# Attention with keys on partitions: row maxima from a first pass put as six rows under the queries

## The chip, the core and the metric

The kernel runs on one core of a Trainium2 chip. The metric is the device time of one execution in microseconds. The engines of a core are TensorE (PE, matrix products into PSUM), VectorE (DVE), ScalarE (ACT), GpSimd (POOL) and SyncE (SP, which issues transfers). Each takes its own instructions in order and they meet only at semaphores.

## The reference

```python
scores = scale * np.matmul(q, k.transpose(0, 1, 3, 2))
scores = np.where(mask, scores, -1000000000.0)
scores = scores - np.max(scores, axis=-1, keepdims=True)
attn = np.exp(scores)
attn = attn / (np.sum(attn, axis=-1, keepdims=True) + 1e-09)
return np.matmul(attn, v).astype(np.float32)
```

There are 2 batches of 8 heads with 768 queries and keys of 64 dimensions, all f32. `mask` is true where a query and a key have the same nearest centroid of 16. The heads' outputs side by side are 1,536 rows of 512, which go through a dense layer pair (512 to 2,048 to 512, with a gate) and then through a top-2 mixture of 8 experts. The change is in the attention part alone.

## The kernel before

Attention takes the first third of the time. The 16 heads (`HEADS`) go in pairs, the middle pairs in a hardware loop, with `x` from 0 to 11 over the pair's tiles of 128 queries (`J` = 6 to a head). For each tile TensorE runs, two tiles ahead, `scores`: 128 queries by 768 keys in two halves of 384 columns, each half a product of the high parts `qa`, `ka` and one of the low parts `qb`, `kb`. Under the 64 dimensions of `qa` and `ka` lie 16 rows that hold the cluster of each query and key, so that the product carries the mask. Two pairs of PSUM banks take the scores in turn. VectorE takes the maximum of a tile (`row_max`), ScalarE the exponential with that maximum as bias (`exps`). The probabilities have queries on partitions, so TensorE transposes them, six blocks of 128 (`turn_probs`), VectorE and ScalarE each copy half of them back (`probs_t`), and `values` multiplies them with the values and a column of ones (`vx`, 65 columns) in plain f32. After six tiles VectorE divides by the denominators (`head_result`, over 6 columns), and after a pair `turn_pair` transposes the result into the layout `xt_hi`, `xt_lo` that the dense layer reads.

Once a head the clusters are found: `similarity` on TensorE, `similarities` and `clusters` on VectorE, `turn_onehot` on TensorE, `cluster_rows` on ScalarE. Bank 7 serves these one after the other (`prep_ready`, `prep_free`). `rows` splits the loaded queries and keys into high and low parts, ScalarE the high and VectorE the low. GpSimd scales the queries and copies the values beside the ones. SyncE loads two heads ahead. What an engine does when is written out by hand in the order of the code. Names of the changed kernel that have a namesake keep its task.

## Time and profile before

| | |
|---|---|
| runs, us | 979.66, 977.3, 978.07 (median 978.07) |
| profiled execution, us | 980.6, of it the span of instructions 978.9 |
| busy, us (share of the span) | PE 928.0 (95%), DVE 535.7 (55%), ACT 407.0 (42%), POOL 115.3 (12%) |
| first product of the dense layers starts at, us | 323.46 |

Matmuls overlap in the pipeline, so the busy time of TensorE says that it has work, not how fast it works; prices are read from distances between starts. A row such as `L719 PE MATMUL psum<-vx,probs_t 128*128 128x65 f32 x12` is twelve records of line 719 with 128x128 weights and 65 moving columns.

### The profile page before, as it was taken

To read this page: it belongs to the slowest core of one execution; us is meant where nothing else is said; L and a number is where in the kernel's file an instruction comes from. 1 tells how busy PE (TensorE), PEld (TensorE's weight loads), DVE (VectorE), ACT (ScalarE), POOL (GpSimd) and SP (SyncE) were. 2 spreads that over 40 slices of the span, in tenths; PEclk is the share of its full clock that TensorE was granted. 3 is DMA by queue.
4 is the path that set the end of the run, shared out by engine and by line. 5 is a ranking of instruction groups with operands and counts; after the bars stand their busy time and mean duration, and the time that the engine had idled before them with its cause. 6 is when DMAs were issued, how large, how long until landed. Compare 5 with 4: busy or idle time off the path is not lost.

```text
span 978.9 us, 15299 instructions
## 1 busy us (share of the span) xinstructions
PE 928.0 (95%) x5483; PEld 826.9 (84%) x5483; DVE 535.7 (55%) x995; ACT 407.0 (42%) x589; POOL 115.3 (12%) x123
## 2 busy tenths in 40 slices
PE   2999999999999999999999996499999999999995
PEld 2999999999999888888888885388888888888884
DVE  4477787787786644355443644254343444435374
ACT  3455665665665522234333422134343342434320
POOL 3010010010010000000500140500000000004162
PEclk9999999999999999999999998599999999999998
DMA  7014214214520522333523342534342634537364
GB/s 208 1 42 125 83 40 123 83 40 123 164 91 1 172 86 100 114 105 113 173 87 127 105 152 86 162 130 154 136 161 86 204 97 153 179 107 244 131 214 156
DMA packets 74052, 118.88 MB, mean 121 GB/s; under 512 B 6970, under 2 KB 37690, under 8 KB 74016
## 3 DMA queue, kind: packets, MB, share of 16 engines
q1 hardware_dynamic: 69088, 104.08, 33.0%
q0 software_dynamic: 4928, 14.35, 4.2%
q8 instruction: 20, 0.33, 0.1%
q14 instruction: 16, 0.13, 0.0%
HBM read 89.12 MB, written 29.39 MB: 121 GB/s over the span
## 4 chain that ended last, share of the span: by engine, by line
PE 94%; DVE 2%; DMA 1%; ACT 1%; POOL 1%; issue 1%; SPq 1%; POOLq 0%; DVEq 0%
PE psum L719 13%; PE psum L777 10%; PE psum L779 10%; PE psum L778 10%; PE psum L791 9%; PE psum L793 9%; PE psum L792 9%; PE psum L709 7%; PE psum L696 4%; PE psum L697 4%; PE psum L925 2%; PE psum L672 2%; PE psum L789 1%; PE psum L788 1%; PE psum L881 1%; PE psum L684 1%
## 5 line engine op out<-in xcount | busy, mean ns | idle before, releaser
L791 PE MATMUL psum<-down_hi,hid_hi 128*128 128x512 f32 x384 | 151.3, 394 | 0.0
L792 PE MATMUL psum<-down_lo,hid_hi 128*128 128x512 f32 x384 | 149.8, 390 | 0.0
L793 PE MATMUL psum<-down_hi,hid_lo 128*128 128x512 f32 x384 | 149.8, 390 | 0.0
L719 PEld LDWEIGHTS psum<-vx,probs_t 128*128 128x128 f32 x1152 | 143.6, 195 | 0.1
L719 PE MATMUL psum<-vx,probs_t 128*128 128x65 f32 x1152 | 141.3, 273 | 0.0
L982 ACT ACTIVATE probs<-psum,neg_max 128x768 f32<-128x768 f32 x96 | 86.5, 901 | 91.6 <-DVE neg_max L1219 91.2
L1114 ACT ACTIVATE hid_hi<-psum 128x448 fp32r<-128x448 f32 x64 | 34.8, 544 | 185.5 <-PE psum L779 185.4
L1474 DVE SCALAR_TENSOR_TENSOR hid_lo<-psum,hid_hi 128x384 fp32r<-128x384 f32 x64 | 35.6, 556 | 123.9 <-ACT hid_hi L1114 123.9
L1219 DVE TENSOR_REDUCE neg_max<-psum 128x1 f32<-128x768 f32 x96 | 91.6, 954 | 16.9 <-PE psum L697 16.9
L777 PE MATMUL psum<-sx_hi,up_hi 128*128 128x448 f32 x256 | 94.7, 370 | 0.0
L778 PE MATMUL psum<-sx_lo,up_hi 128*128 128x448 f32 x256 | 94.4, 369 | 0.0
L779 PE MATMUL psum<-sx_hi,up_lo 128*128 128x448 f32 x256 | 94.3, 368 | 0.0
L1089 ACT ACTIVATE gelu<-psum 128x512 f32<-128x512 f32 x48 | 28.7, 598 | 157.4 <-PE psum L779 157.4
L1242 DVE TENSOR_TENSOR up_lo<-raw,up_hi 128x1024 fp32r<-128x1024 f32 x56 | 68.5, 1223 | 40.6 <-ACT down_hi L1003 40.5
L793 PEld LDWEIGHTS psum<-down_hi,hid_lo 128*128 128x128 f32 x384 | 72.1, 188 | 15.4
L791 PEld LDWEIGHTS psum<-down_hi,hid_hi 128*128 128x128 f32 x384 | 72.1, 188 | 14.6 <-DVE hid_hi L1474 0.2
L709 PE MATMUL psum<-ident,probs 128*128 128x128 f32 x576 | 83.4, 282 | 0.9 <-ACT probs L982 0.7
L792 PEld LDWEIGHTS psum<-down_lo,hid_hi 128*128 128x128 f32 x384 | 72.1, 188 | 13.9
L1258 DVE COPY probs_t<-psum 128x384 f32<-128x384 f32 x96 | 53.3, 555 | 46.6 <-PE psum L709 45.6
L1424 DVE CAST hid_hi<-gelu 128x512 fp32r<-128x512 f32 x48 | 20.8, 432 | 105.5 <-ACT gelu L1089 105.5
L696 PE MATMUL psum<-ka,qa 80*128 80x384 f32 x192 | 75.2, 392 | 1.7 <-ACT ka L977 1.7
L777 PE MATMUL psum<-xt_hi,up_hi 128*128 (+1 forms) x192 | 76.3, 398 | 0.0
(181 smaller groups left out, 1549.1 us busy)
## 6 DMA issues: line engine op xcount, KB each, us to landing
raw<-in_moe_w SPq DMA_DIRECT2D x64, 512.0 KB, 4.3
raw<-in_moe_w_in SPq DMA_DIRECT2D x24, 512.0 KB, 3.4
raw<-in_moe_w_out SPq DMA_DIRECT2D x24, 512.0 KB, 5.1
slot_x<-zeros SPq DMA_DIRECT2D x7, 1024.0 KB, 5.6
raw_q<-in_q SPq DMA_DIRECT2D x32, 192.0 KB, 3.3
raw_k<-in_k SPq DMA_DIRECT2D x32, 192.0 KB, 3.7
slot_rows<-slot_x SPq DMA_DIRECT2D x8, 768.0 KB, 5.4
slot_y<-y_sb SPq DMA_DIRECT2D x7, 768.0 KB, 3.9
```

Of the source, the lines that this page charges most:

```text
L696: mm(dst, qa[0:D + C, s, cols], ka[0:D + C, s, keys], start=True, stop=False)
L709: last = nc.tensor.transpose(psum[:, 4 + half, j * P:(j + 1) * P], src, ident[:])
L719: last = mm(psum[:, 6, i * VW:(i + 1) * VW], probs_t[:, i % 2, j // 3, (j % 3) * P:(j % 3 + 1) * P], vx[:, s, j], start=(j == 0), stop=(j ...
L777: mm(dst, up_hi[:, slot, c, cols], moving_hi(c), start=(c == 0), stop=False)
L778: mm(dst, up_hi[:, slot, c, cols], moving_lo(c), start=False, stop=False)
L779: last = mm(dst, up_lo[:, slot, c, cols], moving_hi(c), start=False, stop=(c == DC - 1))
L791: mm(dst, hid_hi[:, f % 2, cols], down_hi[:, slot, f % GP], start=(f == 0), stop=False)
L792: mm(dst, hid_hi[:, f % 2, cols], down_lo[:, slot, f % GP], start=False, stop=False)
L793: return mm(dst, hid_lo[:, f % 2, cols], down_hi[:, slot, f % GP], start=False, stop=(f == pieces - 1))
L982: copy(probs[:, i % 2].rearrange("p (h n) -> p h n", h=2), src, ACT.Exp, bias=neg_max[:, i % 2:i % 2 + 1]).then_inc(probs_ready, 1)
L1219: dv.tensor_reduce(neg_max[:, i % 2:i % 2 + 1], psum[:, 2 * (i % 2):2 * (i % 2) + 2, 0:HALF], AX.XY, ALU.max, negate=True).then_inc(max_re ...
L1242: dv.tensor_tensor(up_lo[:, slot], raw1[:, stage], up_hi[:, slot].bitcast(F32), ALU.subtract)
```

## The change

The scores of the probabilities are computed with keys on partitions, so that they need no transposing before the product with the values.

- **First pass.** `scores` runs the product of the high parts alone, for one head ahead, into one pair of banks. `row_max` writes the negated maximum of each tile into a column of `neg_max`. After six tiles `turn_max` transposes these columns into 6 rows of 128, and `max_to_rows` writes them as six rows of 768 under the queries of `qa`, each row zero outside its own tile. `ka` has ones in the same six rows, so the second pass subtracts the maximum of each query within the product.
- **Second pass.** A head is 12 units (`UNITS`): two halves of 384 queries, six blocks of 128 keys each. `turned` makes the scores of a unit in two products, two units ahead, in three banks; `exps` takes the exponential; `values` multiplies them in plain f32 with 128 stationary columns, 64 of the values and 64 of ones, and 386 moving columns. Its result has dimensions on partitions for the head's own half and the denominators on the other half.
- **Result.** `denominators` on ScalarE copies the denominators beside the results, `head_result` on VectorE inverts 64 x 384 of them and multiplies, twice a head. `pair_hi` on ScalarE copies that to `xt_hi`, GpSimd subtracts for `xt_lo`. The copies `probs_t`, `turn_probs` and `turn_pair` are gone; so is GpSimd's work on queries and values. The scale is applied in the exponential, the values are loaded in place.
- **Order.** `qa`, `ka`, `qb`, `kb` have three slots, loads are three heads ahead, `raw_q` and `raw_k` one slot. The attention is written out head by head, without loops. The dense layer starts when the first half of the last head is ready.

```diff
-            def load_head(n, s):
+            def load_rows(n):
                 for dst, src in ((raw_q, q_h), (raw_k, k_h)):
                     for half in range(2):
-                        sp.dma_start(dst[half * D:(half + 1) * D, s],
-                                     src[bass.ds(n, 1)].rearrange("o d n -> d (o n)")).then_inc(qk_in[s], DMA)
-                sp.dma_start(raw_v[:, s], v_h[bass.ds(n, 1)].rearrange("o p n -> p (o n)")).then_inc(v_in[s], DMA)
+                        sp.dma_start(dst[half * D:(half + 1) * D], src[n]).then_inc(qk_in, DMA)
+            def load_values(n):
+                sp.dma_start(vx[:, n % 2, :, own(n)], v_h[n]).then_inc(v_in[n % 2], DMA)
...
+            xt_flat = xt_hi[:].rearrange("p c n -> p (c n)"), xt_lo[:].rearrange("p c n -> p (c n)")
+            for n in range(1, HEADS, 2):
+                for half in range(2):
+                    pool.wait_ge(pair_hi_ready, n + half)
+                    hi, lo = (x[:, x_columns(n, half)] for x in xt_flat)
+                    nc.gpsimd.tensor_tensor(lo, head_x[:, half], hi.bitcast(F32), ALU.subtract)\
+                        .then_inc(pair_lo_ready, 1)
...
-            def scores(s, i, u):
+            def scores(m, i):
                 if i == 0:
-                    pe.wait_ge(prep_free, u)
-                p = i % 2
-                cols = slice(i * P, (i + 1) * P)
+                    pe.wait_ge(prep_free, prep[f"turn {m}"] + 1)
+                if m or i:
+                    pe.wait_ge(max_ready, J * m + i)
                 for half in range(2):
-                    keys = slice(half * HALF, (half + 1) * HALF)
-                    dst = psum[:, 2 * p + half, 0:HALF]
-                    mm(dst, qa[0:D + C, s, cols], ka[0:D + C, s, keys], start=True, stop=False)
-                    last = mm(dst, qb[:, s, cols], kb[:, s, keys], start=False, stop=True)
+                    last = mm(psum[:, half, 0:HALF], qa[0:D + C, m % SLOTS, i * P:(i + 1) * P],
+                              ka[0:D + C, m % SLOTS, half * HALF:(half + 1) * HALF], start=True, stop=True)
                 last.then_inc(scores_ready, 1)
...
+            def turn_max(m, use, tiles):
+                pe.wait_ge(max_ready, J * m + tiles)
+                pe.wait_ge(prep_free, prep[use])
+                nc.tensor.transpose(psum[0:J, 7, 0:P], neg_max[:, m % 2], ident[:]).then_inc(prep_ready, 1)
+            def turned(n, u, rows_set=None):
+                half, c = divmod(u, J)
+                at = UNITS * n + u
+                if rows_set is not None:
+                    pe.wait_ge(max_rows, rows_set)
+                if at >= SLOTS:
+                    pe.wait_ge(probs_ready, at - SLOTS + 1)
+                dst = bank(2 + at % SLOTS)[:, 0:HALF]
+                keys, queries = slice(c * P, (c + 1) * P), slice(half * HALF, (half + 1) * HALF)
+                mm(dst, ka[0:ROWS, n % SLOTS, keys], qa[0:ROWS, n % SLOTS, queries], start=True, stop=False)
+                mm(dst, kb[:, n % SLOTS, keys], qb[:, n % SLOTS, queries], start=False, stop=True)\
+                    .then_inc(turned_scores, 1)
+            def values(n, u):
+                half, c = divmod(u, J)
+                at = UNITS * n + u
+                if u == 0:
+                    pe.wait_ge(v_in[n % 2], DMA * (n // 2 + 1))
+                if c == 0 and n:
+                    pe.wait_ge(head_out, 2 * (n - 1) + half + 1)
+                pe.wait_ge(probs_ready, at + 1)
+                mm(psum[:, 5 + half, 0:WIDE], vx[:, n % 2, c], probs[:, at % SLOTS], start=(c == 0),
+                   stop=(c == J - 1)).then_inc(unit_done, 1)
+            def ahead(n, u):
+                if u + 2 < UNITS:
+                    turned(n, u + 2, 2 if n == 0 and u + 2 == J else None)
+                elif n + 1 < HEADS:
+                    turned(n + 1, u + 2 - UNITS, n + 3 if u + 2 == UNITS else None)
...
+            def head(n):
+                for u in range(UNITS):
+                    ahead(n, u)
+                    values(n, u)
+                    if n + 1 < HEADS:
+                        if u in (0, 2, 4, 6):
+                            scores(n + 1, 2 + u // 2)
+                        elif u == 8:
+                            turn_max(n + 1, f"max {n + 1}", J)
+                    if n + 2 < HEADS:
+                        if u == 1:
+                            similarity(n + 2)
+                        elif u == 5:
+                            turn_onehot(n + 2)
+                        elif u in (8, 10):
+                            scores(n + 2, (u - 8) // 2)
...
+            def exps(n, u):
+                at = UNITS * n + u
+                act.wait_ge(turned_scores, at + 1)
+                if at >= SLOTS:
+                    act.wait_ge(unit_done, at - SLOTS + 1)
+                copy(probs[:, at % SLOTS, 0:HALF], psum[:, 2 + at % SLOTS, 0:HALF], ACT.Exp, scale=float(D) ** -0.5)\
+                    .then_inc(probs_ready, 1)
+            def denominators(n, half):
+                act.wait_ge(unit_done, UNITS * n + (half + 1) * J)
+                if n:
+                    act.wait_ge(head_out, 2 * (n - 1) + half + 1)
+                copy(recip[own(n), half], psum[other(n), 5 + half, 0:HALF], ACT.Copy, bias=1e-9)\
+                    .then_inc(denom_ready, 1)
...
-            def row_max(tile, i):
-                dve.wait_ge(scores_ready, tile + 1)
-                dv.tensor_reduce(neg_max[:, i % 2:i % 2 + 1], psum[:, 2 * (i % 2):2 * (i % 2) + 2, 0:HALF],
-                                 AX.XY, ALU.max, negate=True).then_inc(max_ready, 1)
-            def head_result(n, s, chain):
-                dve.wait_ge(pv_done, J * n + J)
-                o = psum[:, 6, 0:J * VW].rearrange("p (j w) -> p j w", w=VW)
-                chain.link(dv.tensor_scalar(denom[:], o[:, :, D:VW], 1e-9, None, ALU.add))
-                chain.link(dv.reciprocal(recip[:], denom[:]))
-                dv.tensor_tensor(pair_x[:, :, s * D:(s + 1) * D], o[:, :, 0:D], recip[:].broadcast_to((P, J, D)),
-                                 ALU.mult).then_inc(head_out, 1)
-            def pair_lo(g, half):
-                dve.wait_ge(pair_hi_ready, 2 * g + half + 1)
-                at = (g & (DC - 1)) * N + (g & DC) * (S // DC) + half * HALF
-                hi = xt_hi[:].rearrange("p c n -> p (c n)")[:, bass.ds(at, HALF)].bitcast(F32)
-                lo = xt_lo[:].rearrange("p c n -> p (c n)")[:, bass.ds(at, HALF)]
-                dv.tensor_tensor(lo, psum[:, 7, 0:HALF], hi, ALU.subtract).then_inc(prep_free, 1)
+            def row_max(m, i):
+                dve.wait_ge(scores_ready, J * m + i + 1)
+                dv.tensor_reduce(neg_max[:, m % 2, i:i + 1], psum[:, 0:2, 0:HALF], AX.XY, ALU.max, negate=True)\
+                    .then_inc(max_ready, 1)
...
+            def max_to_rows(m, use, first, count):
+                full = (J, count, P)
+                dve.wait_ge(prep_ready, prep[use] + 1)
+                dv.scalar_tensor_tensor(
+                    out=qa[TOP:ROWS, m % SLOTS, first * P:(first + count) * P].rearrange("r (j q) -> r j q", q=P),
+                    in0=psum[0:J, 7, 0:P].rearrange("r (o q) -> r o q", o=1).broadcast_to(full), scalar=LARGEST,
+                    in1=own_tile[0:J, first:first + count].rearrange("r (j o) -> r j o", o=1).broadcast_to(full),
+                    op0=ALU.min, op1=ALU.mult).then_inc(prep_free, 1)
+                dve.wait_ge(prep_free, prep[use] + 1)
+                dve.sem_inc(max_rows, 1)
+            def head_result(n, half):
+                rows, held = own(n), psum[own(n), 5 + half]
+                dve.wait_ge(denom_ready, 2 * n + half + 1)
+                if n >= 2:
+                    dve.wait_ge(pair_lo_ready, 2 * (n // 2 - 1) + half + 1)
+                chain.mark(dv.tensor_scalar(mean_v[rows, half:half + 1], held[:, HALF:HALF + 1], 1e-9 / S, None,
+                                            ALU.mult))
+                chain.link(dv.reciprocal(recip[rows, half], recip[rows, half]))
+                dv.scalar_tensor_tensor(out=head_x[rows, half], in0=held[:, 0:HALF], scalar=mean_v[rows, half:half + 1],
+                                        in1=recip[rows, half], op0=ALU.add, op1=ALU.mult).then_inc(head_out, 1)
...
+            def head(n):
+                if n + 2 < HEADS:
+                    rows(n + 2, 1)
+                if n + 1 < HEADS:
+                    row_max(n + 1, 2)
+                head_result(n - 1, 1)
+                if n + 2 < HEADS:
+                    similarities(n + 2)
+                if n + 1 < HEADS:
+                    row_max(n + 1, 3)
+                if n + 2 < HEADS:
+                    clusters(n + 2)
+                if n + 1 < HEADS:
+                    row_max(n + 1, 4)
+                    row_max(n + 1, 5)
+                head_result(n, 0)
+                if n + 1 < HEADS:
+                    max_to_rows(n + 1, f"max {n + 1}", 0, J)
+                if n + 2 < HEADS:
+                    row_max(n + 2, 0)
+                    row_max(n + 2, 1)
+                if n + 3 < HEADS:
+                    rows(n + 3, 0)
...
+            pe.wait_ge(pair_lo_ready, PAIRS)
+            pe.wait_ge(head_out, 2 * HEADS - 1)
+            chunk(0, None)
+            pe.wait_ge(pair_lo_ready, 2 * PAIRS)
```

The next two pieces are VectorE's order, first of a head in the loop of the kernel before, from the result of the head before it. `neg_max` is the maximum of a tile, `probs_t` the copy of its transposed half; lines 1210 to 1214 are `clusters`.

```order
L1225 TENSOR_SCALAR denom<-psum 128x6
L69 ISA
L1226 RECIPROCAL recip<-denom 128x6
L69 REGISTER_ALU
L1227 TENSOR_TENSOR pair_x<-psum,recip 128x6x64
L1201 ISA
L1203 TENSOR_REDUCE sim<-psum 128x192
L1257 ISA
L1258 COPY probs_t<-psum 128x384
L1218 REGISTER_ALU
L1219 TENSOR_REDUCE neg_max<-psum 128x1
```

In the changed kernel the same engine between the clusters of one head and the second result of that head, from `row_max` of tiles 4 and 5 on:

```order
L1294 TENSOR_REDUCE neg_max<-psum 128x1 x2
L1315 TENSOR_SCALAR mean_v<-psum 64x1
L1317 RECIPROCAL recip<-recip 64x384
L1318 SCALAR_TENSOR_TENSOR head_x<-psum,mean_v,recip 64x384
L1301 SCALAR_TENSOR_TENSOR qa<-psum,own_tile 6x768
L1294 TENSOR_REDUCE neg_max<-psum 128x1 x2
L1268 SCALAR_TENSOR_TENSOR qb<-qa,split_q,raw_q 128x768
L1268 SCALAR_TENSOR_TENSOR kb<-ka,split_k,raw_k 128x768
L1294 TENSOR_REDUCE neg_max<-psum 128x1
```

The result of a head stands twice in a head instead of once, with 384 columns instead of 6, and ahead of the six rows of maxima; the copies are gone.

On TensorE a tile of the kernel before reads (transposes of the probabilities, scores two tiles ahead, values of the tile before):

```order
L709 MATMUL psum<-ident,probs 128x128 x6
L696 MATMUL psum<-ka,qa 128x384
L697 MATMUL psum<-kb,qb 128x384
L696 MATMUL psum<-ka,qa 128x384
L697 MATMUL psum<-kb,qb 128x384
L719 MATMUL psum<-vx,probs_t 128x65 x6
```

and in the changed kernel units 8 to 10 of a head, with the scores of the first pass (line 707) between them; the product of line 727 at unit 10 is the first that reads the six rows:

```order
L727 MATMUL psum<-qa,ka 128x384
L728 MATMUL psum<-qb,kb 128x384
L740 MATMUL psum<-probs,vx 128x386
L715 MATMUL psum<-ident,neg_max 6x128
L707 MATMUL psum<-ka,qa 128x384 x2
L727 MATMUL psum<-qa,ka 128x384
L728 MATMUL psum<-qb,kb 128x384
L740 MATMUL psum<-probs,vx 128x386
L727 MATMUL psum<-qa,ka 128x384
L728 MATMUL psum<-qb,kb 128x384
L740 MATMUL psum<-probs,vx 128x386
L707 MATMUL psum<-ka,qa 128x384 x2
```

The six transposes and their products of 65 columns are replaced by one product of 386 columns a unit, and `neg_max` is turned between unit 8 and 9.

## Rows read from the trace of the kernel before

**Rows 1.** The page, part 4, shares of the chain that ended last.

```profile
PE 94%; DVE 2%; DMA 1%; ACT 1%; POOL 1%; issue 1%; SPq 1%; POOLq 0%; DVEq 0%
```

**Rows 2.** TensorE in order of time, 199 to 238 us: start, duration, line, names, form.

```profile
199.79 0.82 PE L672 MATMUL psum<-cen_r,qb 128*128 x6
...
220.57 1.45 PE L719 MATMUL psum<-vx,probs_t 128*128 128x65 f32 x12
221.85 0.82 PE L709 MATMUL psum<-ident,probs 128*128 128x128 f32 x6
222.43 0.42 PE L696 MATMUL psum<-ka,qa 80*128 80x384 f32 x1
222.69 0.34 PE L697 MATMUL psum<-kb,qb 128*128 128x384 f32 x1
222.87 0.34 PE L696 MATMUL psum<-ka,qa 80*128 80x384 f32 x1
...
224.60 0.62 PE L684 MATMUL psum<-ident_b,onehot 128*16 128x128 bf16 x12
...
236.48 0.82 PE L672 MATMUL psum<-cen_r,qb 128*128 x6
237.15 0.82 PE L672 MATMUL psum<-cen_r,kb 128*128 x6
```

**Rows 3.** All engines in order of time, the start of the attention part.

```profile
21.89 0.69 PE L696 MATMUL psum<-ka,qa 80*128 80x384 f32 x1 [1.71 <-ACT ka L977]
...
22.70 0.52 PE L696 MATMUL psum<-ka,qa 80*128 80x384 f32 x1
23.02 0.52 PE L697 MATMUL psum<-kb,qb 128*128 128x384 f32 x1
...
23.57 0.96 DVE L1219 TENSOR_REDUCE neg_max<-psum 128x1 f32<-128x768 f32 x1 [4.44 <-PE psum L697]
...
43.25 0.34 PE L697 MATMUL psum<-kb,qb 128*128 128x384 f32 x1
43.43 0.34 PE L696 MATMUL psum<-ka,qa 80*128 80x384 f32 x1
```

**Rows 4.** Groups of VectorE by line and form: busy us, mean ns, idle before.

```profile
L1219 DVE TENSOR_REDUCE neg_max<-psum 128x1 f32<-128x768 f32 x96 | 91.6, 954 | 16.9 <-PE psum L697 16.9
...
L1242 DVE TENSOR_TENSOR up_lo<-raw,up_hi 128x1024 fp32r<-128x1024 f32 x56 | 68.5, 1223 | 40.6 <-ACT down_hi L1003 40.5
...
L1258 DVE COPY probs_t<-psum 128x384 f32<-128x384 f32 x96 | 53.3, 555 | 46.6 <-PE psum L709 45.6
...
L1197 DVE SCALAR_TENSOR_TENSOR qb<-qa,split_q,raw_q 128x768 fp32r<-128x768 f32 x16 | 16.2, 1010 | 3.4 <-ACT qa L968 3.4
...
L1214 DVE TENSOR_TENSOR onehot<-iota_c,first_hit 128x192 bf16<-128x192 f32 x16 | 6.7, 420 | 0.6
...
L1213 DVE TENSOR_REDUCE first_hit<-hit 128x12 f32<-128x192 f32 x16 | 5.6, 353 | 0.6
```

**Rows 5.** Single lines of VectorE: ns min/median/max, first and last start.

```profile
L1184 DVE RECIPROCAL cen_s<-cen_s x1: 164/164/164, 6.0 to 6.0; 128x1 f32<-128x1 f32 x1
...
L1382 DVE RECIPROCAL r_t<-r_t x3: 178/178/178, 465.7 to 610.1; 128x4 f32<-128x4 f32 x3
...
L1226 DVE RECIPROCAL recip<-denom x16: 191/192/192, 53.4 to 323.9; 128x6 f32<-128x6 f32 x16
...
L1225 DVE TENSOR_SCALAR denom<-psum x16: 164/164/165, 53.2 to 323.7; 128x6 f32<-128x6 f32 x16
```

**Rows 6.** Two lines of TensorE with plain f32 products, same columns.

```profile
L719 PE MATMUL psum<-vx,probs_t x1152: 219/275/418, 33.2 to 323.4; 128*128 128x65 f32 x192
...
L881 PE MATMUL psum<-wr,yt x96: 177/263/263, 420.0 to 602.5; 128*128 128x16 f32 x96
```

**Rows 7.** Groups of ScalarE by line and form.

```profile
L1016 ACT ACTIVATE probs_t<-psum 128x384 f32<-128x384 f32 x96 | 46.5, 485 | 18.3 <-PE psum L709 18.1
...
L977 ACT ACTIVATE ka<-psum 16x768 fp32r<-16x768 bf16 x16 | 12.9, 803 | 0.2
```

More of the change, by code:

```diff
@@ L32 @@
 MASKED = 1e30
+LARGEST = 1e25
 CAP = 448
@@ L327, in rows_of @@
             return P if j < FULL else REST
-        def unit(g, k, first=False):
-            return 2 + k if first and k < 2 else 6 * g + k
+        prep = {}
+        for use in ("sim 0", "turn 0", "max 0", "max 0 again", "sim 1", "turn 1", "sim 2", "turn 2", "max 1"):
+            prep[use] = len(prep)
+        for n in range(1, HEADS):
+            for use, m in (("sim", n + 2), ("turn", n + 2), ("max", n + 1)):
+                if m < HEADS:
+                    prep[f"{use} {m}"] = len(prep)
         AT_LOGITS = TPC
@@ L767, in up @@
+            similarity(0)
+            turn_onehot(0)
+            for i in range(J // 2):
+                scores(0, i)
+            turn_max(0, "max 0", J // 2)
+            turned(0, 0, 1)
+            turned(0, 1)
+            for i in range(J // 2, J):
+                scores(0, i)
+            turn_max(0, "max 0 again", J)
+            first_head()
+            for n in range(1, HEADS):
+                head(n)
             def up(f, slot, moving_hi, moving_lo, width, group, turned_in=None):
@@ L1033, in _, with next_exps @@
[L1033 to L1043 removed]
+            def next_exps(n, u):
+                if u + 1 < UNITS:
+                    exps(n, u + 1)
+                elif n + 1 < HEADS:
+                    exps(n + 1, 0)
@@ L1044, in take_y @@
+            rows(0, 0)
+            rows(0, 1)
+            cluster_rows(0)
+            rows(1, 0)
+            rows(1, 1)
+            exps(0, 0)
+            first_head()
+            for n in range(1, HEADS):
+                head(n)
+            denominators(HEADS - 1, 1)
             def take_y(first):
@@ L1276, in _ @@
-            for n in range(2):
-                for w in range(2):
-                    rows(n, n, w)
-            similarities(0)
-            clusters(chain, 0)
-            row_max(0, 0)
-            row_max(1, 1)
-            pair(0, True, False, chain)
-            before_pairs = chain.n
-            PER_PAIR = 2 * 4 + 2 * 2
-            with dve.Fori(1, PAIRS - 1) as g:
-                body = Tally(dve, dve_chain, before_pairs + (g - 1) * PER_PAIR)
-                pair(g, False, False, body)
-                assert body.n == PER_PAIR
@@ L1290, in _, with first_head @@
-            chain = Tally(dve, dve_chain, before_pairs + (PAIRS - 2) * PER_PAIR)
-            pair(PAIRS - 1, False, True, chain)
-            head_result(HEADS - 1, 1, chain)
-            split(0, 1, 0)
-            split(0, 1, 1)
+            def first_head():
+                rows(1, 0)
+                rows(1, 1)
+                similarities(1)
+                clusters(1)
+                rows(2, 0)
+                rows(2, 1)
+                row_max(1, 0)
+                row_max(1, 1)
+                similarities(2)
+                row_max(1, 2)
+                clusters(2)
+                row_max(1, 3)
+                head_result(0, 0)
+                row_max(1, 4)
+                row_max(1, 5)
+                max_to_rows(1, "max 1", 0, J)
+                row_max(2, 0)
+                row_max(2, 1)
+                rows(3, 0)
@@ new lines, in _ @@
+            rows(0, 0)
+            rows(0, 1)
+            similarities(0)
+            clusters(0)
+            for i in range(J // 2):
+                row_max(0, i)
+            max_to_rows(0, "max 0", 0, J // 2)
+            for i in range(J // 2, J):
+                row_max(0, i)
+            max_to_rows(0, "max 0 again", J // 2, J // 2)
+            first_head()
+            for n in range(1, HEADS):
+                head(n)
+            for x in range(4):
+                split(0, x // 2, x % 2)
```

366 lines of the change are left out of this document (153 added, 213 removed).

## Prediction

> **What bounds the kernel now.** I read the chain of waits first. TensorE holds 94% of the chain that ended last [rows 1], so the question is what it issues in the attention part and whether anything stops it there. In the time-ordered rows of TensorE the same place of the loop (the two similarity groups) comes at 199.79 and at 236.48 us: a pair of heads takes 36.69 us, a head 18.35 us, and between those points TensorE stands without a gap [rows 2]. The reader should take prices from the distance of starts, because the durations overlap: six transposes of the probabilities 0.58 us (221.85 to 222.43), a product of 384 columns 0.18 us (222.69 to 222.87) or 0.26 us where it follows transposes (222.43 to 222.69), twelve value records 1.28 us (220.57 to 221.85), a similarity group of six 0.67 us (236.48 to 237.15), the twelve one-hot transposes about 0.6 us. A tile of 128 queries is then 0.58 + 0.26 + 3 x 0.18 + 1.28 = 2.66 us, and six tiles, 1.34 of similarity, 0.6 of one-hot and 0.33 of pair transposes make 18.2 of the 18.35 us. VectorE works beside it: per tile 0.954 us of maximum and a copy of 0.555 us [rows 4]. It has about 4 us of slack in a head.
>
> At the start products of 384 columns stand 0.32 us apart (22.70 to 23.02), and 0.18 us apart from 43.25 us on [rows 3]: 384 columns in 0.32 us are 1.2 GHz, so the tiles before that run at the lower clock and the rest at 2.4 GHz; I go by these distances, since the clock row of the page shows no drop there. The six value tiles of head 0 are done at 53.2 us, those of head 15 at 323.7 [rows 5].
>
> **What the change does to TensorE.** Per head it removes 36 transposes (6 x 0.58 = 3.5 us), 72 value records (6 x 1.28 = 7.7 us), half of the 24 score products of the first pass, and the pair transposes. It adds 12 units, each of two products of 384 columns (0.36 us) and one product of 386 columns in plain f32. The trace shows no wide f32 product. It does show that an f32 product is two records (1,152 for 576), and the shortest record goes from 177 ns at 16 columns to 219 at 65 [rows 6]: 42/49 = 0.86 ns a column, twice the 0.42 that one column takes at 2.4 GHz. So I take 386 x 0.86 = 0.33, with a little for issue 0.34 us a record and 0.67 a unit. From below, one record could cost 0.18 like the 384-column row; from above I allow double, 0.68. A unit is 0.36 + 0.67 = 1.03 us, and a head 12 x 1.03 + 12 x 0.18 (first pass) + 1.34 + 0.6 + 0.1 (turning the maxima) = 16.6 us. On TensorE alone the change gives 1.75 us a head.
>
> **What it does to VectorE.** Per head: six maxima 6 x 0.954 = 5.7 us, two splits of rows 2.0, sim 0.56, clusters 4 x 0.353 + 0.42 = 1.8, and no copies of probabilities any more [rows 4]. New is `max_to_rows`, six partitions by 768 elements: 1.0 us, like the 768-element row split. New too are two results a head: a tensor_scalar 0.16, a reciprocal over 64 x 384, and a multiplication of 384 columns 0.56, priced like the copy. The reciprocal is the disputed price. Before, it ran over 6 columns. Its three rows are 164 ns for 1 column, 178 for 4, 192 for 6, while the tensor_scalar of 6 columns takes 164 [rows 5]. End to end that is 28/5 = 5.6 ns a column, where ordinary operations pay about 1.05 (555 ns for 384, 954 for 768 [rows 4]). Over 384 columns: 0.16 + 383 x 0.0056 = 2.3 us. From below, if only the fixed part differs, 0.56 us as an ordinary operation of 384 columns; from above the steepest pair of rows, 7 ns: 2.84 us. I take 2.3, since sixteen repeats of the 6-column row spread by 1 ns. VectorE then has 5.7 + 2.0 + 0.56 + 1.8 + 1.0 + 2 x (0.16 + 2.3 + 0.56) = 17.1 us a head, over TensorE's 16.6.
>
> The Trainium skill, "VectorE: DVE Perf Modes", in the walkthrough of the 8-slice pipeline, says that a reciprocal is an iterated divide with a repeat count of 8. If that is 8 cycles a column at the page's 0.96 GHz, an estimate from that page is 3.35 us, and the sum below would end near 1,033 us; the three rows, 14 ns apart each, are flatter than that.
>
> **The ring of waits.** The two engines wait for each other, so I walked one head, with t = 0 where `max_to_rows` ends and about 0.05 us for each hand-over. TensorE stands at unit 10, whose first product reads those rows. It issues the unit (1.1 us, first product 0.26) and then `scores` of tile 1, which needs `row_max` 0 (done at 1.0): the scores are there at 1.8 (the last product runs 0.34 after its start). VectorE waits from 1.0 to 1.8, takes `row_max` 1 to 2.75, the row splits to 3.7 and 4.6, `row_max` 2 to 5.5, `head_result` of the previous half to 8.4, sim to 8.9, `row_max` 3 to 9.7, `clusters` to 11.6. TensorE, past its units 11 and 0 to 5, waits 0.4 us for the one-hot, turns it until 12.2, issues unit 6 and the scores of tile 5, done at 13.9. There is one pair of banks for the first pass, so VectorE waits from 12.5 (after `row_max` 4) to 13.9; that is the largest wait. `row_max` 5 ends at 14.9. ScalarE's cluster rows (2 x 0.8), one exponential and the denominator copy (0.485 each [rows 7]) end at 14.85, just in time. `head_result` takes 14.9 to 17.8, `max_to_rows` to 18.75. TensorE has reached unit 10 at about 17 and waits 1.7 us. Queued behind that waiting product are the values of unit 10 and the scores of the next head, which VectorE waits for: the ring closes at **18.75 us a head against 18.35**. ScalarE has 15 operations of 384 columns and 4 of 768 a head, 15 x 0.485 + 4 x 0.8 = 10.5 us [rows 7], and only queues.
>
> **The ends.** Start: scores of head 0 can begin at 21.9 as before [rows 3], since the longer chain of constants on VectorE takes back what the missing scaling on GpSimd gives. But then six times (scores 1.0 at the low clock, maximum 0.95) run one after the other, where before two buffers let tiles overlap; with two turns of the maxima, 1.0 us each, and two units between, unit 0 begins near 37 us. Head 0 holds two similarities, two clusterings and a result, with 1.93 us a unit until the clock rises near 55: the first `max_to_rows` of a full ring ends at 68.4, and head 0's twelve units at 70.9, against 53.2 before: +17.7. Thirteen rings: 13 x (18.75 - 18.35) = +5.2. End: head 14 without clusters needs 17.1 from ring to ring, then 2.5 + 12 x 1.03 = 14.9 to the last value at 68.4 + 243.75 + 17.1 + 14.9 = 344.2. VectorE has its last full result at 343.4 and two weight splits of 1.22 [rows 4] behind it, so the first layer starts at 345.8 instead of 323.46 and loses 1.0 in its second piece to the last `head_result`; it saves 0.65 of pair transposes. In all +22.7 us. The rest of the kernel moves as a block. The profiled execution took 980.6 (span 978.9): 1,003.3, and scaled to the median of the runs, 978.07/980.6, **1,001 us**.
>
> How it hangs on the reciprocal: 26 of them in the rings, one in head 0 and four at the end lie in the chain, so 0.1 us of its price is 3.1 us of the kernel. The sum breaks even at 2.3 - 22.7/31 = 1.57 us.
>
> **Rivals.** (1) *Cheap reciprocal, TensorE stays the bound; faster.* At 0.56 us VectorE has 13.6 us a head and the ring follows TensorE with about 16.8: 66.6 + 13 x 16.8 + 14.3 + 14.9 = 314.2, the first layer 9 us earlier in all: about 969. For it: the 10 ns between tensor_scalar and reciprocal at few columns might be fixed. Against it: 164, 178 and 192 rise with the columns. It decides for faster below 1.57 us. (2) *Steeper reciprocal:* 2.84 us gives 1,018; the pair 4 to 6 columns speaks for it, 1 to 4 against. The count of 8 in the Trainium skill's page (above) points the same way and further. (3) *The scores' hand-over is looser than my walk* (VectorE's next operation can begin some 0.08 before the last ends, and both engines may settle with less than 2.2 us of VectorE waiting): 1 us less in a ring is 985. (4) *Values at 0.68 us a record:* a unit of 1.7, a head of 24.7 on TensorE, 13 x 6 more, about 1,085. The 0.86 ns a column speaks against it. (5) *The ends alone:* if the clock rose during the first maxima, head 0 would be some 6 us shorter, 995; this lies in the forecast's own range and its chance in the forecast's.
>
> **How the numbers follow.** Forecast (reciprocal 2.0 to 2.6, own range 990 to 1,012): 0.46. Rival 1: 0.18. Rival 2: 0.17. Rival 3, 975 to 990: 0.16, of which a little falls under 978. Rival 4: 0.03. Range 971 to 1,030: left out are most of rival 1 and rival 4. About 0.3% is what a measurement of this kernel can tell from no change. Faster 0.20, within 0.04, slower 0.76.
>
> **What would show it.** In the changed profile: RECIPROCAL 64x384 near 2,300 ns (under 1,500 my sign is wrong); value records at starts 0.34 us apart; TensorE idle some 2 us a head, ended by the `max_to_rows` and `onehot` of VectorE, where it had none; VectorE idle before `row_max` on the scores product; equal places 18.75 us apart; unit 0 of head 0 near 37 us and the first layer near 346 us. I'd be wrong if TensorE showed no such waits, or if the exponentials of ScalarE were what values wait for.

## The result, and the profile after

The changed kernel takes 1031.61 us (median of 4 runs, 1028.8 to 1033.08) against 977.84 us before (4 runs). The ratio is 1.055, with a 95% interval of 1.0533 to 1.0567. The profiled execution took 1033.1 us. The forecast was 1,001 with a range of 971 to 1,030: the direction was right, the size less than half of what was measured.

The page of the changed kernel, its busy times, shares of the chain and costliest groups, beside [rows 1] and [rows 4]:

```profile
PE 929.2 (90%) x4300; PEld 747.4 (72%) x4300; DVE 583.7 (57%) x953; ACT 387.9 (38%) x621; POOL 98.9 (10%) x109
...
PE 71%; DVE 20%; issue 4%; ACT 2%; DMA 1%; POOL 1%; POOLq 0%; DVEq 0%; SPq 0%; ACTq 0%
...
L740 PE MATMUL psum<-probs,vx 128*128 128x386 f32 x384 | 171.0, 529 | 5.0 <-ACT probs L1018 5.0
...
L1294 DVE TENSOR_REDUCE neg_max<-psum 128x1 f32<-128x768 f32 x96 | 91.6, 954 | 65.5 <-PE psum L707 63.5
...
L727 PE MATMUL psum<-qa,ka 102*128 102x384 f32 x192 | 93.1, 485 | 31.5 <-DVEq L1307 31.5
...
L1317 DVE RECIPROCAL recip<-recip 64x384 f32<-64x384 f32 x32 | 81.4, 2542 | 0.5
```

TensorE's share of the chain fell from 94% to 71%, VectorE's rose from 2% to 20%. Before, TensorE waited 1.7 us in all for other engines ahead of its score products (`idle before` of line 696); now line 727 alone waits 31.5 us for line 1307, which is the signal behind `max_to_rows`, and VectorE's maxima wait 63.5 us for the scores (16.9 before, [rows 4]). The two engines wait for each other. The reciprocal is 2,542 ns.

One ring of the changed kernel in order of time, from the maxima of tiles 4 and 5 to the first values of the next ring (columns as in [rows 3]):

```profile
205.22 0.36 DVE L1288 TENSOR_TENSOR onehot<-iota_c,first_hit 128x192 bf16<-128x192 f32 x1
205.50 0.95 DVE L1294 TENSOR_REDUCE neg_max<-psum 128x1 f32<-128x768 f32 x1
205.64 0.64 PE L697 MATMUL psum<-ident_b,onehot 128*32 128x128 bf16 x12 [0.20 <-DVE onehot L1288]
...
207.87 0.96 DVE L1294 TENSOR_REDUCE neg_max<-psum 128x1 f32<-128x768 f32 x1 [1.41 <-PE psum L707]
...
208.98 0.16 DVE L1315 TENSOR_SCALAR mean_v<-psum 64x1 f32<-64x1 f32 x1 [0.16 <-ACT recip L1026]
209.18 2.55 DVE L1317 RECIPROCAL recip<-recip 64x384 f32<-64x384 f32 x1
...
210.50 0.81 PE L740 MATMUL psum<-probs,vx 128*128 128x386 f32 x2
211.76 0.62 DVE L1318 SCALAR_TENSOR_TENSOR head_x<-psum,mean_v,recip 64x384 f32<-64x384 f32 x1
212.42 0.95 DVE L1301 SCALAR_TENSOR_TENSOR qa<-psum,own_tile 6x768 fp32r<-6x768 f32 x1
...
213.48 0.44 PE L727 MATMUL psum<-qa,ka 102*128 102x384 f32 x1 [2.17 <-DVEq L1307]
...
215.09 0.53 PE L727 MATMUL psum<-qa,ka 102*128 102x384 f32 x1
215.33 0.96 DVE L1294 TENSOR_REDUCE neg_max<-psum 128x1 f32<-128x768 f32 x1 [0.86 <-PE psum L707]
215.41 0.53 PE L728 MATMUL psum<-qb,kb 128*128 128x384 f32 x1
215.73 1.49 PE L740 MATMUL psum<-probs,vx 128*128 128x386 f32 x2
```

Follow the brackets: VectorE waits 1.41 us for the scores of tile 5, ScalarE's denominators come 0.16 us after the maximum, then reciprocal, product and six rows run one after the other while TensorE, done with unit 9, waits 2.17 us. That is the ring as forecast. What the forecast didn't have is in the last lines: two products that stand 0.18 us apart at full clock (the prediction's price) stand 0.32 us apart at 215.09 and 215.41. TensorE runs at 1.2 GHz again. Short windows around the wait, which ends at 213.48, show the granted clock at half of full speed from 214.8 us on, while TensorE is busy throughout (columns: window, its length, busy time of TensorE with its instructions, granted clock, share and rate of the transfers):

```profile
211.00:213.40 2.40, 0.31 (x1) 1.00 0.00 0
213.40:214.80 1.40, 1.32 (x5) 1.00 0.00 0
214.80:217.80 3.00, 3.00 (x9) 0.50 0.00 0
```

The same engine in stretches from one `max_to_rows` to the next, with the same columns:

```profile
87.37:108.55 21.18, 18.59 (x85) 0.92 0.31 96
108.55:128.15 19.60, 17.00 (x85) 1.00 0.19 51
128.15:149.32 21.17, 18.57 (x85) 0.92 0.32 97
149.32:168.92 19.60, 17.00 (x85) 1.00 0.20 51
168.92:190.11 21.19, 18.61 (x85) 0.92 0.33 97
190.11:212.42 22.31, 19.93 (x85) 0.85 0.18 45
```

A ring is 19.60 us where the granted clock is 1.00, 21.2 where it is 0.92, 22.3 where it is 0.85. In nine of the thirteen rings from 87 to 356 us the clock is below 1.00: in all seven that begin with a wait of 2.17 to 2.19 us, and in two of the six that begin with one of 2.03 to 2.05. (The first expectation below counts 8 of 13; it is nine.) In all nine the low stretch begins between 0.2 us before the end of that wait and 1.4 us after it. The ring before these, the first full one, takes 23.43 us at a granted clock of 0.85.

### The profile page after: what moved, and what is told of

It reads as the page before. It is cut to its first block, busy times and chain, and to the rows that moved or that the text cites. A ratio compares the mean times of both kernels' runs of the same rounds, so it can differ in the third digit from the quotient of the medians.

```text
span 1031.3 us, 12264 instructions
## 1 busy us (share of the span) xinstructions
PE 929.2 (90%) x4300; PEld 747.4 (72%) x4300; DVE 583.7 (57%) x953; ACT 387.9 (38%) x621; POOL 98.9 (10%) x109
## 3 DMA queue, kind: packets, MB, share of 16 engines
q1 hardware_dynamic: 79328, 104.08, 31.5%
## 4 chain that ended last, share of the span: by engine, by line
PE 71%; DVE 20%; issue 4%; ACT 2%; DMA 1%; POOL 1%; POOLq 0%; DVEq 0%; SPq 0%; ACTq 0%
PE psum L812 10%; PE psum L813 9%; PE psum L814 9%; PE psum L826 9%; PE psum L827 8%; PE psum L828 8%; DVE recip L1317 7%; PE psum L740 4%; DVE neg_max L1294 3%; PE psum L957 2%; PE psum L707 2%; DVE head_x L1318 2%; PE psum L727 2%; DVE qa L1301 2%; PE psum L824 1%
## 5 line engine op out<-in xcount | busy, mean ns | idle before, releaser
L740 PE MATMUL psum<-probs,vx 128*128 128x386 f32 x384 | 171.0, 529 | 5.0 <-ACT probs L1018 5.0
L1018 ACT ACTIVATE probs<-psum 128x384 f32<-128x384 f32 x192 | 90.9, 489 | 113.2 <-PE psum L728 111.6
L1294 DVE TENSOR_REDUCE neg_max<-psum 128x1 f32<-128x768 f32 x96 | 91.6, 954 | 65.5 <-PE psum L707 63.5
L727 PE MATMUL psum<-qa,ka 102*128 102x384 f32 x192 | 93.1, 485 | 31.5 <-DVEq L1307 31.5
L707 PE MATMUL psum<-ka,qa 80*128 80x384 f32 x192 | 79.1, 496 | 9.9 <-DVE neg_max L1294 8.1
L826 PEld LDWEIGHTS psum<-down_hi,hid_hi 128*128 128x128 f32 x384 | 72.1, 188 | 14.7 <-DVE hid_hi L1576 0.2
L740 PEld LDWEIGHTS psum<-probs,vx 128*128 128x128 f32 x384 | 76.5, 207 | 8.1 <-ACT probs L1018 7.9
L1317 DVE RECIPROCAL recip<-recip 64x384 f32<-64x384 f32 x32 | 81.4, 2542 | 0.5
```

What stands on the lines that cost most here:

```text
L707: last = mm(psum[:, half, 0:HALF], qa[0:D + C, m % SLOTS, i * P:(i + 1) * P], ka[0:D + C, m % SLOTS, half * HALF:(half + 1) * HALF], start ...
L727: mm(dst, ka[0:ROWS, n % SLOTS, keys], qa[0:ROWS, n % SLOTS, queries], start=True, stop=False)
L740: mm(psum[:, 5 + half, 0:WIDE], vx[:, n % 2, c], probs[:, at % SLOTS], start=(c == 0), stop=(c == J - 1)).then_inc(unit_done, 1)
L826: mm(dst, hid_hi[:, f % 2, cols], down_hi[:, slot, f % GP], start=(f == 0), stop=False)
L1018: copy(probs[:, at % SLOTS, 0:HALF], psum[:, 2 + at % SLOTS, 0:HALF], ACT.Exp, scale=float(D) ** -0.5)\
L1294: dv.tensor_reduce(neg_max[:, m % 2, i:i + 1], psum[:, 0:2, 0:HALF], AX.XY, ALU.max, negate=True)\
```

## The experiments

All are edits of the changed kernel or of the experiment named. Ratios are to the kernel before, whose medians beside them were 977.9 and 977.5 us.

**No reciprocal.** The reciprocal becomes a multiplication by one, so attention's output is left multiplied by its denominators.

```diff
-                chain.link(dv.reciprocal(recip[rows, half], recip[rows, half]))
+                chain.link(dv.tensor_scalar(recip[rows, half], recip[rows, half], 1.0, None, ALU.mult))
```

> The changed kernel with the reciprocal of 64 x 384 replaced by a multiplication by 1.0 of the same shape, so the outputs of attention are multiplied by their denominators instead of divided. Theory (ring): the 2.54 us of each reciprocal lie in a ring of waits between VectorE and TensorE, and TensorE's wait of some 2.1 us at unit 10 is also what lowers its granted clock in 8 of 13 rings. Then the ring falls from a mean of 20.9 us to about 17.0, every ring has granted clock 1.00, the waits on the max rows are under 0.5 us and the time is 975 us (965 to 985). Rival 1 (the clock falls for another reason, such as the mix of products): rings of 17 plus about 1.3 us from the lower clock, 992. Rival 2 (the reciprocal runs beside TensorE and costs nothing): 1,025 or more.

The time of the whole, 1,940.7 us, says nothing: the wrong attention output changes what the router does, and the experts run two to three times as many products (768 of line 826 against 384, 768 of line 812 with `sx_hi` against 256). The attention part can be read. From here on the rings are distances between the starts of `max_to_rows`: 16.5 to 16.7 us from the second on, and the first layer starts at 309.84 instead of 375.19, 65.4 us sooner, which for the whole would be 966 us. Both rivals fall: after the first ring TensorE no longer waits for the six rows, the granted clock of the stretch is 0.99, and 31 reciprocals of 2.54 us (one of 0.35 each in their place) give 68 us.

**Useless products in the wait.** Sixteen products of 128 columns before the wait at unit 10, and in a later run eight.

```diff
-                if rows_set is not None:
-                    pe.wait_ge(max_rows, rows_set)
                 if at >= SLOTS:
...
+                if rows_set is not None:
+                    if n > 1:
+                        for x in range(FILL):
+                            mm(dst[:, 0:P], kb[:, (n - 1) % SLOTS, 0:P], qb[:, (n - 1) % SLOTS, 0:P],
+                               start=True, stop=True)
+                    pe.wait_ge(max_rows, rows_set)
```

> The changed kernel with 16 useless products of 128 columns put ahead of the first product of unit 10, in front of its wait for the max rows (heads 2 to 15), into the bank that this product overwrites. They fill some 1.8 of the 2.1 us in which TensorE stands. Theory (standing still lowers the clock): granted clock 1.00 in nearly every ring, rings of 19.6 to 19.8 us throughout, time 1,014 us (1,010 to 1,020), faster with more work. Rival (the low clock has another cause, or comes in a fixed rhythm): rings as before at a mean of 20.9 or more, 1,031 to 1,036.

> As the changed kernel with useless products before the wait at unit 10, but 8 of them instead of 16, so that TensorE works for 0.9 us and then stands for some 1.2 us. Theory (the clock falls after a long standstill, and waits of 1.2 us in a row of another experiment left it at 1.00): rings of 19.6 to 20.0 us and 1,018 us as with 16. Rival (each wait lowers the clock in proportion): half of the gain, about 1,025. Rival 2 (the gain with 16 came from something else in these products): anything else.

With 16 the median is 1018.31 us (ratio 1.0412, 1.0367 to 1.0457), with 8 it is 1019.29 (1.042, 1.0389 to 1.0452): 13 and 12 us less than without, with more work. Windows of the kernel with 8, as above:

```profile
87.55:107.51 19.96, 17.88 (x93) 1.00 0.35 103
107.51:127.11 19.60, 17.89 (x93) 1.00 0.21 50
127.11:147.08 19.97, 17.88 (x93) 1.00 0.33 103
```

And two waits of TensorE in it, in order of time:

```profile
148.14 0.44 PE L732 MATMUL psum<-qa,ka 102*128 102x384 f32 x1 [1.19 <-DVEq L1312]
...
167.72 0.44 PE L732 MATMUL psum<-qa,ka 102*128 102x384 f32 x1 [1.32 <-DVEq L1312]
```

and its ScalarE, earlier:

```profile
97.45 0.52 ACT L1037 ACTIVATE xt_hi<-head_x 128x384 fp32r<-128x384 f32 x1 [3.94 <-DVE head_x L1323]
```

Granted clock 1.00 in every ring after the first, which has no filler (0.85 there in both runs). In these rings waits of 1.2 to 1.3 us leave the clock alone; those of 2.17 to 2.19 always lower it in the changed kernel. That holds for one wait in a ring: the first ring of the run of eight is at 0.85 after four waits of 1.05 to 1.64 us within 8 us. A filler both shortens the standstill and adds work, and the two runs don't tell which of these keeps the clock. The rings are 19.96 and 19.60 in turn, in both runs: the products fit in the standstill and cost nothing. The 0.36 us of every other ring come by way of ScalarE: its copy `xt_hi` waits 3.94 us for the second result of the head before, three exponentials are queued behind it, and TensorE waits 0.70 us for the first of them. The rival of a loss in proportion to the wait falls with the run of eight: it is not at 1,025 us.

**1/d on ScalarE.** Two operations of ScalarE take the place of its copy and of VectorE's reciprocal. The kernel leaves out the 1e-9 beside the denominators.

```diff
-                copy(recip[own(n), half], psum[other(n), 5 + half, 0:HALF], ACT.Copy, bias=1e-9)\
-                    .then_inc(denom_ready, 1)
+                at = 2 * n + half
+                copy(recip[own(n), half], psum[other(n), 5 + half, 0:HALF], ACT.Ln).then_inc(log_ready, 1)
+                act.wait_ge(log_ready, at + 1)
+                copy(recip[own(n), half], recip[own(n), half], ACT.Exp, scale=-1.0).then_inc(denom_ready, 1)
...
+            nc.scalar.preload_act_table_set(EXP_AND_LN)
...
-                chain.link(dv.reciprocal(recip[rows, half], recip[rows, half]))
```

> The changed kernel with 1/d made on ScalarE as exp(-ln d): the copy of the denominators becomes a logarithm, and an exponential follows; VectorE has no reciprocal of 64 x 384 any more (the 1e-9 beside d is left out). One table set holds both functions and is loaded once. Theory (ring): VectorE loses 5.1 us a head, ScalarE gains 1.0 us; the ring is then TensorE's own 16.8 to 17.2 us with one short wait, granted clock 1.00, time 978 us (968 to 988), about level with the kernel before. Rival 1 (ScalarE becomes what ends the wait, since its queue already ends just in time): rings of 18 or more, 993 or more. Rival 2 (the reciprocal is no part of the ring): 1,025 or more.

968.62 us, ratio 0.9904 (0.9875 to 0.9932): 1% faster than the kernel before, with an interval clear of 1, and 9 us under what I expected, inside the range. The rings are 16.79 to 16.83 us from the second on, at a granted clock of 1.00. Its trace, at the same place of a ring:

```profile
213.63 0.48 ACT L1028 ACTIVATE recip<-psum 64x384 f32<-64x384 f32 x1
214.15 0.52 ACT L1030 ACTIVATE recip<-recip 64x384 f32<-64x384 f32 x1
214.70 0.16 DVE L1319 TENSOR_SCALAR mean_v<-psum 64x1 f32<-64x1 f32 x1 [0.72 <-ACT recip L1030]
214.90 0.62 DVE L1321 SCALAR_TENSOR_TENSOR head_x<-psum,mean_v,recip 64x384 f32<-64x384 f32 x1
215.55 0.95 DVE L1305 SCALAR_TENSOR_TENSOR qa<-psum,own_tile 6x768 fp32r<-6x768 f32 x1
...
216.61 0.44 PE L728 MATMUL psum<-qa,ka 102*128 102x384 f32 x1 [0.16 <-DVEq L1311]
```

ScalarE adds 0.52 us to the path where VectorE took 2.54, and TensorE's wait shrinks from 2.17 to 0.16 us. The rival that ScalarE becomes the one that is waited for shows in its 0.72 us before `mean_v`, but little of this reaches TensorE.

**Another order on VectorE.** The six rows and one maximum ahead of the first result of the head.

```diff
-                head_result(n, 0)
                 if n + 1 < HEADS:
                     max_to_rows(n + 1, f"max {n + 1}", 0, J)
                 if n + 2 < HEADS:
                     row_max(n + 2, 0)
+                head_result(n, 0)
+                if n + 2 < HEADS:
                     row_max(n + 2, 1)
```

> The changed kernel with VectorE's order changed alone: in every head from 1 on the six max rows and the first maximum of the next head come ahead of the first result of the head instead of behind it. No operation is added or removed. Theory (it is the place of the reciprocal in the ring, not VectorE's total, that makes TensorE wait at unit 10): TensorE no longer waits 2.1 us there but about 0.5 us at the first values of the next head; ring 18.6 to 18.8 us, granted clock 1.00, time 1,002 us (996 to 1,012). Rival 1 (the wait moves whole to the next values product): ring 19.6 with or without the low clock, 1,014 to 1,031. Rival 2 (VectorE's total of 17.8 us a head is the bound): ring 17.8, 990.

1035.06 us, ratio 1.0585 (1.0539 to 1.0631), not faster than the changed kernel: this expectation failed, and the time lies above both rivals too. The rings are 22.2 to 22.9 us after odd heads and 19.5 after even ones. The trace shows two things that my walk had left out. After odd heads ScalarE stands 5.65 us in front of its copy `xt_hi`, which waits for the late result, with the exponential of unit 11 queued behind, and TensorE waits for that:

```profile
210.78 0.95 DVE L1301 SCALAR_TENSOR_TENSOR qa<-psum,own_tile 6x768 fp32r<-6x768 f32 x1 [1.15 <-PE psum L715]
...
216.30 0.52 ACT L1032 ACTIVATE xt_hi<-head_x 128x384 fp32r<-128x384 f32 x1 [5.65 <-DVE head_x L1318]
216.73 0.47 ACT L1018 ACTIVATE probs<-psum 128x384 f32<-128x384 f32 x1
...
217.25 1.66 PE L740 MATMUL psum<-probs,vx 128*128 128x386 f32 x2 [3.40 <-ACT probs L1018]
```

And in the first line VectorE itself now waits 1.15 us for the turned maxima, which TensorE issues only behind the values of unit 8. Where the reciprocal came first, it covered that time.

**The same order, with the copy out of the way.** ScalarE's `xt_hi` of the first half moves from unit 9 to unit 1 of the next head.

```diff
+                    elif u == 1 and n % 2 == 0:
+                        pair_hi(n - 1, 0)
...
-                    elif u == 9 and n % 2 == 1:
-                        pair_hi(n, 0)
```

> The kernel with the max rows ahead of the first result, and besides ScalarE's copy of that result into xt_hi moved from unit 9 of the head to unit 1 of the next, so that the exponentials of unit 11 do not queue behind it. Theory (in odd heads the exponentials stood behind the copy, which waited for the late result): odd rings fall from 22.6 to about 19.5 us, granted clock 1.00 throughout, time about 1,012 us (1,006 to 1,018). If the order itself were a gain as I had walked it, rings of 18.7 and 1,002. Rival (the wait of values for the late result remains and lowers the clock all the same): 1,022 or more.

1025.22 us, ratio 1.0473 (1.0439 to 1.0507). The waits of 3.4 us are gone, but the expectation of 1,012 is missed by 13 us. Windows from one `max_to_rows` to the next:

```profile
127.52:148.66 21.14, 18.81 (x87) 0.92 0.33 97
148.66:168.19 19.53, 17.47 (x87) 1.00 0.21 51
168.19:189.16 20.97, 17.53 (x87) 1.00 0.32 98
...
289.65:312.40 22.75, 20.41 (x87) 0.85 0.30 90
```

Two waits of TensorE in the same trace:

```profile
153.98 0.89 PE L740 MATMUL psum<-probs,vx 128*128 128x386 f32 x2 [1.23 <-issue]
...
173.78 0.89 PE L740 MATMUL psum<-probs,vx 128*128 128x386 f32 x2 [1.50 <-issue]
```

A ring is 19.53 or 20.97 at full clock, against 19.60 and 19.96 in the kernels with useless products: not shorter in the mean than without the new order. TensorE's wait has moved to the first values of the next head, which need the late result (the view says `issue`, but `head_x` ends at 153.88 and the values start at 153.98). From 85 us on the six rings with a wait of 1.23 us are at 1.00 throughout; of the seven with one of 1.50 us four are at 1.00 (as the one of 20.97 above) and three below it. In two of these three the low stretch begins only 4.4 and 6.1 us after that wait, with a wait of 0.77 or 0.78 us between, so that the wait of 1.50 us is not shown to be its cause. Neither of the two orders tried makes a ring shorter; only taking the reciprocal out of VectorE did.

**What a column costs.** Each reciprocal in four pieces with the same result.

```diff
-                chain.link(dv.reciprocal(recip[rows, half], recip[rows, half]))
+                first = 0
+                for width in (24, 72, 96, 192):
+                    piece = recip[rows, half, first:first + width]
+                    chain.link(dv.reciprocal(piece, piece))
+                    first += width
```

> The changed kernel with each reciprocal of 64 x 384 cut into four of 24, 72, 96 and 192 columns; the result is the same. It measures what a column of a reciprocal costs. If the price is linear from the first column, as the three short rows of the kernel before and the 2.54 us at 384 columns suggest (6.2 ns a column beside 0.16 us fixed), the four take 306, 604, 753 and 1,348 ns. If instead a column costs more after some width (the 14 ns between rows of 4 and 6 columns), the short ones lie below that line: 24 columns under 280 ns. Four fixed parts and hand-overs add about 0.55 us twice a head, so the time is near 1,031 + 28 x 0.55 = 1,046.

Groups of VectorE between 60 and 330 us (columns as in [rows 4]):

```profile
L1320 DVE RECIPROCAL recip<-recip 64x192 f32<-64x192 f32 x25 | 33.7, 1347 | 0.9
L1320 DVE RECIPROCAL recip<-recip 64x96 f32<-64x96 f32 x24 | 17.9, 747 | 0.8
L1320 DVE RECIPROCAL recip<-recip 64x72 f32<-64x72 f32 x24 | 14.3, 597 | 0.8
L1320 DVE RECIPROCAL recip<-recip 64x24 f32<-64x24 f32 x24 | 7.0, 292 | 0.4
```

From 24 to 192 columns that is (1,347 - 292)/168 = 6.28 ns a column, and 141 ns fixed; 384 columns on this line are 2.55 us. The price is linear, and the rival of a cheaper short piece falls (24 columns take 292 ns, not under 280). Six columns would be 180 ns where [rows 5] have 192: the shortest rows lie a little above the line, which is why a slope between them comes out too flat. The one run took 1054.66 us, 9 more than expected, at a granted clock of 0.952 over the kernel. It also bounds what the wait says of the clock. TensorE waits 2.56 to 2.74 us in each of its thirteen rings from the second on, longer than in the changed kernel; ten are below 1.00 and three at 1.00, this one among them:

```profile
219.37:240.43 21.06, 17.04 (x85) 1.00 0.32 98
...
220.43 0.44 PE L727 MATMUL psum<-qa,ka 102*128 102x384 f32 x1 [2.74 <-DVEq L1307]
```

So a long wait often lowers the clock and does not always.

**The start.** On top of the kernel with 1/d on ScalarE, the first pass of head 0 in two pairs of banks in turn.

```diff
+        def first_bank(m, i):
+
+            return 5 if m == 0 and i % 2 else 0
...
-                if m or i:
-                    pe.wait_ge(max_ready, J * m + i)
+                if m or i > 1:
+                    pe.wait_ge(max_ready, J * m + i - (m == 0))
```

> The kernel with 1/d on ScalarE as exp(-ln d), and besides head 0's first pass in two pairs of PSUM banks in turn (0 and 1, 5 and 6) instead of one. Theory (the start is a serial chain of six times scores and maximum, 2.06 us each): scores hide behind maxima, unit 0 of head 0 starts some 4 us sooner than 36.9, time 4 us less than the 968.6 of the kernel without this, 965 (962 to 967). Rival (the time saved is given back in head 0, whose similarity waits for VectorE's row splits, and the products run at the lower clock for as long): under 1 us, 968.

964.28 us, ratio 0.9855 (0.9831 to 0.988), 4.3 us less than without. The values of unit 0, with one pair of banks (the changed kernel) and with two:

```profile
36.92 1.49 PE L740 MATMUL psum<-probs,vx 128*128 128x386 f32 x2
```

```profile
32.81 1.49 PE L745 MATMUL psum<-probs,vx 128*128 128x386 f32 x2
```

4.1 us sooner, and none of it is given back. The first layer starts 5.2 us sooner than with 1/d on ScalarE alone (307.08 against 312.29): the first full ring is now at a granted clock of 1.00 and 18.26 us, where it was at 0.91 and 19.19. This is the fastest version measured, 13 us under the kernel before.

## Why the prediction was wrong in size

**Right: the ring and its place.** Head by head the trace follows the walk: VectorE's wait for the scores of tile 5 (1.4 forecast, 1.41), the denominators just in time (0.16), the wait of TensorE at unit 10 before the six rows (1.7 forecast, 2.03 to 2.17). Without the reciprocal it is gone. Unit 0 of head 0 at 36.9 us was forecast "near 37". TensorE alone was forecast at 16.6 us a head and is 16.8 in the kernel with 1/d on ScalarE; the value records were taken as 0.34 us apart in that sum and stand 0.32 apart. Their price, worked out of two shortest records [rows 6], held.

**Wrong: the step that left TensorE at full clock.** The sum priced every ring after the first at 2.4 GHz and counted the wait at unit 10 as lost time alone. The runs showed that the wait of 2.1 us also lowers the granted clock, to 0.92 or 0.85 of a ring's mean. The first layer begins at 375.19 us against 345.8 forecast, 29.4 us late, and filling the wait with useless products brings it to 360.47: 14.7 of the 29.4 us. The fillers don't stand in the first full ring, which is at 0.85 in both fill runs as well, so the whole of the clock's part is larger. In the kernel before there was nothing to see of this in the attention part, as TensorE never stood there once it had begun; it stood at the start of the experts, where the page's clock row falls, and I didn't read that row for this purpose.

**Mis-sized: the reciprocal.** 2.3 us in the sum, 2.54 measured. With 31 of them in the chain, 0.24 x 31 = 7.4 us. That is within the forecast's own condition (2.0 to 2.6) and would have given about 1,008 us, so it alone doesn't explain the miss. The Trainium skill ("VectorE: DVE Perf Modes", the walkthrough of the 8-slice pipeline) has a repeat count of 8, from which the estimate was 3.35 us; the runs say 6.28 ns a column, which is nearer to the rows of this case, and the measurement decides. That the sum by this estimate, 1,033 us, falls beside the measured 1,031.6 is luck: its price is 0.8 us too high for each of 31 reciprocals, and the low clock and the longer rings make up for it.

**Mis-sized: the rest of a ring.** At full clock and with the measured reciprocal the walk gives 18.75 + 2 x 0.24 = 19.2 us, the rings with fillers are 19.8 in the mean. The product behind the reciprocal takes 0.617 instead of 0.56 us, 0.12 a ring; 0.18 a ring are the exponentials behind ScalarE's copy; the last 0.25 are what is left over, and I put them to hand-overs without having measured them. That is 0.55 x 12 = 6.6 us.

**The whole of it.** The kernel with sixteen fillers still reaches the first layer 14.7 us later than forecast (360.47 against 345.8), and by place these are: head 0, 3.8 us quicker (its first `max_to_rows` of a full ring ends at 64.6, not at 68.4); the first ring, 23.5 us where 19.2 are due, +4.3, of which some 3 us are the granted clock of 0.85 (an estimate: later rings at 0.85 take 22.3 us against 19.6); 26 reciprocals in the rings, +6.2; the rest of twelve rings, +6.6; the two last heads with their four reciprocals, +1.4. With the 14.7 us that the fillers give back this makes the 29.4. So the low clock is some 18 of the 29.4 us.

**The rivals.** That the reciprocal is cheap and the kernel faster: wrong, though its consequence, a TensorE-bound attention of 16.8 us a head and 969 us, was met by the kernel that has no reciprocal on VectorE (968.6); that is another kernel, and no credit to this rival. The steeper reciprocal (1,018) was the nearest of the forecasts, for a part of the reason. The looser hand-over went the other way. The break-even of 1.57 us wasn't tried at that value.

## What to carry to other kernels

Where two engines hand work to each other in a ring, write the ring out, since neither engine's busy share (57% for VectorE here) shows it; and look in it for the one operation whose price was read at another width. Reckon a wait of TensorE of 2 us or more twice: the time itself, and what the clock often loses after it (here 1.6 or 2.7 us). Such a ring is mended by making the long operation short or giving it to a third engine that has slack, not by another order, as far as two tries show: the first queued exponentials behind a copy, and the second moved the wait to the next product in line.

## What the runs showed of the hardware

A reciprocal on VectorE costs 6.28 ns a column beside 0.14 us fixed (24 to 384 columns, f32, 64 partitions), six times the 1.05 ns of an ordinary operation [rows 4]. ScalarE's logarithm and exponential of 384 columns cost 485 and 521 ns.

TensorE's granted clock, by ring from the second on, with the wait at the six rows or, in the two other orders, at the values that wait longest:

| kernel | wait, us | rings below 1.00 |
|---|---|---|
| six rows first | 3.39 to 3.41 | 7 of 7 |
| reciprocal in four pieces | 2.56 to 2.74 | 10 of 13 |
| changed kernel | 2.17 to 2.19 | 7 of 7 |
| changed kernel | 2.03 to 2.05 | 2 of 6 |
| copy out of the way | 1.50 to 1.51 | 3 of 7 |
| both other orders | 1.22 to 1.24 | 0 of 12 |
| eight fillers | 1.19 to 1.33 | 0 of 13 |
| sixteen fillers | up to 0.45 | 0 of 13 |

In the changed kernel the low clock made a ring 1.6 us longer (21.2 against 19.6) or 2.7 (22.3). Some of these rings hold further waits of up to 1.3 us, the last one of a kernel often one of 1.6 to 2.3. Several waits close together lower the clock too: the first full ring, about whose start lie three or four of mostly 1.05 to 1.64 us, was at 0.84 to 0.91 in every kernel but the one with two pairs of banks at the start, where it was at 1.00. Why equal waits sometimes keep the clock and sometimes not isn't settled.
